# Loading and pooling kv in 8 KB rows with parts of a band matrix, and ten unread products as TensorE's first work

## The chip, the cores and the metric

The kernel runs on one core of a Trainium2 chip. The metric is device time in microseconds (us) of one execution; lower is better. Before the change it takes 1547.98 us, the median of 3 runs (1547.93 to 1549.79).

## What is computed

Three parts follow one another: an attention whose keys and values are a pooled picture, and two feed-forward layers. All data is float32.

```python
B, C, Hh, Ww = (1, 128, 384, 32)             # q: [1, 12288, 128], kv: [1, 384, 32, 128]
kv_pool = kv.reshape(B, H // 4, 4, W // 4, 4, C).mean(axis=(2, 4))
kv_flat = kv_pool.reshape(B, -1, C) @ w_sr   # 768 keys of 128 numbers
k = v = kv_flat
s = (q @ k.transpose(0, 2, 1)) / np.sqrt(C)
a = np.exp(s - s.max(-1, keepdims=True))
a /= a.sum(-1, keepdims=True) + 1e-09
x = (a @ v)
h = x @ w_in1;  x = (np.maximum(h, 0) + alpha * np.minimum(h, 0)) @ w_out1
h = x @ w_in2;  P = a0 + a1*h + a2*h**2 + a3*h**3
Q = 1.0 + abs(b0) * abs(h) + abs(b1) * h**2
out = (P / (Q + 1e-06)) @ w_out2
```

The order of the 768 keys does not matter, as long as keys and values have the same one.

## The kernel before

The work falls into three stages: the **load phase** (kv is loaded and pooled, keys and values are made), the **attention** (24 groups of 512 queries), and the two **layers** (24 groups, 16 blocks of 128 hidden numbers each). Every engine has a program of its own, written out by hand in a fixed order; semaphores tie them together.

**Load phase.** The keys are made in 6 chunks of 128. For each chunk SyncE's queue (SP, L197) issues 4 DMAs of 256 KB. `kv_rows` (L47) puts one 4 x 4 cell of the picture, which is one key, on each partition; of each of its 4 picture rows a partition gets 4 pixels x 128 numbers, that is 2 KB in one piece. A chunk is 16 pixels x 128 numbers on each of the 128 partitions. VectorE sums the first 8 pixels of a chunk (`pool_keys`, one reduction L907 of 1024 numbers to 128 on each partition) as soon as the first two DMAs have landed. TensorE adds up the other 8 pixels by 8 products with the identity (L1363), whose result stands transposed in PSUM, and then adds VectorE's sum with a ninth (L1365). In float32 each such product is recorded as 2 instructions. ScalarE copies the chunk out, divided by 16 (`copy_pooled_t`, L431); TensorE multiplies it with w_sr (`key_chunk`, L1372, and for each three chunks the values, L1376). Two such halves of 384 keys are then split in a high and a low part, by ScalarE (`keys_hi` L437, `values_hi` L442) and VectorE (`keys_lo` L915, `values_lo` L954). The attention's first scores (L1345) wait for the second `keys_lo`.

Between these, TensorE transposes the queries of the first two groups (`queries`, L1404), ScalarE and VectorE split them (`query_hi` L468, `query_lo` L948). After kv, SP issues w_in1 (L199, 1 MB in rows of 8 KB) and w_out1 (L200, 1 MB in pieces of 512 B), and then the queries of each further group when `qt_ready` says that a buffer is free; after three of these it issues w_in2 (L206, 1 MB in rows of 8 KB), which stands in the notes of the profile as in_moe_w_in too.

ScalarE's queue issues at the start w_sr, alpha (8 KB), the coefficients a and b (L423, L424, each given to all 128 partitions, 16 and 8 bytes per partition) and the queries of the first two groups (L426). ScalarE then makes abs(b) (L462). VectorE makes 1 - alpha (L944) after its first reduction, and waits for abs(b) before it. TensorE's first instruction is the transpose of alpha (L1352).

**Attention.** In each step TensorE runs the scores of one group, the transposes of its probabilities and the products with the values (`tile_scores`, `transposed`, `weighted`).

**Entry to the layers.** ScalarE's last piece of the attention is `attended_hi` (L496). It then loads two coefficients into registers and starts `negative(0, 0)` (L552), for whose end TensorE waits with its third block of the first layer.

Of the kernel before, what the change touches and what calls it, by code (L numbers as in the profile page):

```python
# [9 lines left out]
ALU = mybir.AluOpType  # L10
# [3 lines left out]
P = 128  # L14
# [19 lines left out]
def build(nc, q, kv, w_sr, w_in1, w_out1, alpha, w_in2, w_out2, coef_p, coef_q, out):  # L34
# [12 lines left out]
    kv_rows = kv[0].rearrange("(hh r) (ww x) c -> hh ww r (x c)", r=POOL_SIDE, x=POOL_SIDE)  # L47
    key_rows = P // kv_rows.shape[1]
# [4 lines left out]
    with ctx:  # L53
# [48 lines left out]
        pooled = early[:, 0:keys].rearrange("p (c n) -> p c n", c=CHUNKS)  # L102
        w_sr_sb = early[:, keys:keys + P]
        al_rows = early[0:BLOCKS, keys + P:keys + 2 * P]
# [9 lines left out]
        DVE_PIXELS, POOLED, VALUES = 2 * POOL_SIDE, (2, 3, 5, 6, 7, 2), (3, 6)  # L114
# [5 lines left out]
        for name in (  # L120

            *(f"ld_kv{c}{part}" for c in range(CHUNKS) for part in "ab"), "ld_wsr", "ld_in1", "ld_out1", "ld_in2", "ld_out2", "ld_al", "ld_ab", "ld_q0", "ld_q1", "st_out",
# [70 lines left out]
        def _(sp):  # L193

            for c in range(CHUNKS):
                for r in range(POOL_SIDE):
                    sp.dma_start(kv_in[:, c, r * POOL_SIDE * P:(r + 1) * POOL_SIDE * P],  # L197
                                 kv_rows[c * key_rows:(c + 1) * key_rows, :, r, :]).then_inc(s[f"ld_kv{c}{'aabb'[r]}"], 16)
            sp.dma_start(raw_in[0], w_in1).then_inc(s["ld_in1"], 16)  # L199
            sp.dma_start(wout1[:], w_out1.rearrange("(b p) c -> p b c", p=P)).then_inc(s["ld_out1"], 16)  # L200
            for g in range(GROUPS - 2):
                sp.wait_ge(s["qt_ready"], g + 1)
                sp.dma_start(q_in[:, g % 2, :], q_groups[g + 2]).then_inc(s[f"ld_q{g % 2}"], 16)
                if g == 2:
# [213 lines left out]
        def _(act):  # L418
# [122 lines left out]
            act.wait_ge(s["cols_done"], 1)  # L541
# [361 lines left out]
        def _(dve):  # L903
            def pool_keys(c):

                dve.wait_ge(s[f"ld_kv{c}a"], 32)
                nc.vector.tensor_reduce(pooled[:, c, :],  # L907
                                        kv_in[:, c, 0:DVE_PIXELS * P].rearrange("p (j c) -> p c j", j=DVE_PIXELS),
                                        AX.X, ALU.add).then_inc(s["pooled_done"], 1)
# [31 lines left out]
            dve.wait_ge(s["ld_ab"], 32)
            dve.wait_ge(s["absb_col_done"], 1)
            dve.wait_ge(s["al_ready"], 1)
            nc.vector.tensor_scalar(one_minus_al[:], banks[:, 7, 0:BLOCKS], -1.0, 1.0, ALU.mult, ALU.add).then_inc(s["cols_done"], 1)  # L944
# [56 lines left out]
            for g in range(STEPS):  # L1001
# [340 lines left out]
        def _(pe):  # L1342
# [6 lines left out]
            pe.wait_ge(s["ident_ready"], 1)  # L1349

            pe.wait_ge(s["ld_al"], 16)
            nc.tensor.transpose(banks[:, 7, 0:BLOCKS], al_rows, ident[0:BLOCKS, 0:BLOCKS]).then_inc(s["al_ready"], 1)  # L1352

            def pooled_transpose(c):

                dst = banks[:, POOLED[c], 0:P]
# [4 lines left out]
                pe.wait_ge(s[f"ld_kv{c}b"], 32)  # L1361
# [411 lines left out]
```

## Time and profile before

| | us |
|---|---|
| median of 3 runs | 1547.98 |
| the profiled execution | 1547.8 |
| span of its records | 1546.0 |
| TensorE busy, of the span | 1508.4 (98%) |
| VectorE busy | 1433.9 (93%) |
| ScalarE busy | 1401.4 (91%) |
| GpSimd busy | 1230.5 (80%) |

The profiled execution lies 0.2 us under the median of the runs, and 1.8 us of it lie outside the span. PE is TensorE's matmul side, PEld its loading of weights, DVE VectorE, ACT ScalarE, POOL GpSimd, SP SyncE. A "releaser" is what ended an engine's idle time. Times in rows are counted from the start of the span. In the DMA share, 1.00 means that all 16 DMA engines are busy.

### The profile page before, as it was taken

The numbers are of one execution on the slowest core, as the hardware profiler recorded it, in microseconds if no ns is written. First come the engines' busy times: TensorE is split into PE (matmuls) and PEld (weight loads), VectorE is DVE, ScalarE is ACT, GpSimd is POOL, SyncE is SP. The second block draws the span as 40 slices with busy tenths as digits, with TensorE's granted clock in tenths as the row PEclk, the third lists the DMA queues.
The fourth block names the chain that finished last, engine by engine and source line by source line (L and its number), as shares of the span: only waits on it lengthen the run. The fifth ranks groups of instructions, "written<-read, shape, count | busy, mean of one in ns | idle before, by whom it ended". The sixth has DMA issues, their size and how long they took to land. (4 is left out here: it accounts for less than half of the span.)

```text
span 1546.0 us, 28282 instructions
## 1 busy us (share of the span) xinstructions
PE 1508.4 (98%) x8269; PEld 1247.6 (81%) x8269; DVE 1433.9 (93%) x2260; ACT 1401.4 (91%) x2714; POOL 1230.5 (80%) x1346
## 2 busy tenths in 40 slices
PE   6999999999999999999999999999999999999986
PEld 5899999867888888888888888888888888888875
DVE  4788888739999999999999999999999999999998
ACT  1677777749999999999999999999999999999997
POOL 0444444408999999999999999999999999999997
PEclk9999999999999999999999999999999999999998
DMA  8100010000000000000000000000000000000000
GB/s 247 54 24 22 29 48 21 1 1 1 8 8 1 8 8 8 8 1 8 8 8 1 8 8 8 8 1 8 8 8 1 8 8 8 8 1 8 8 8 8
DMA packets 12330, 24.94 MB, mean 16 GB/s; under 512 B 1536, under 2 KB 1680, under 8 KB 11920
## 3 DMA queue, kind: packets, MB, share of 16 engines
q1 hardware_dynamic: 11424, 22.55, 4.7%
q8 instruction: 65, 1.06, 0.3%
q14 instruction: 89, 0.73, 0.1%
q10 hardware_dynamic: 752, 0.60, 0.1%
HBM read 16.85 MB, written 6.29 MB: 15 GB/s over the span
## 5 line engine op out<-in xcount | busy, mean ns | idle before, releaser
L285 POOL TENSOR_TENSOR cubic<-sq,lin_p 128x512 f32<-128x512 f32 x384 | 495.1, 1289 | 75.1 <-ACT sq L560 48.5
L276 POOL TENSOR_TENSOR rational<-newton,ratio 128x512 f32<-128x512 f32 x333 | 429.7, 1291 | 30.8 <-PE banks L1544 21.3
L1544 PEld LDWEIGHTS banks<-wout,rational 128*128 128x128 f32 x3072 | 403.0, 194 | 41.1 <-issue 10.6
L1544 PE MATMUL banks<-wout,rational 128*128 128x128 f32 x3072 | 405.4, 277 | 1.9 <-POOL rational L276 1.4
L1345 PE MATMUL banks<-x_hi,win_lo 128*128 128x512 f32 x768 | 387.8, 505 | 15.0 <-DVE ratio L1054 12.6
L1347 PE MATMUL banks<-x_hi,win_hi 128*128 128x512 f32 x768 | 303.3, 395 | 0.0
L1346 PE MATMUL banks<-x_lo,win_hi 128*128 128x512 f32 x768 | 302.6, 394 | 0.0
L578 ACT ACTIVATE lin_p<-banks,ab_raw 128x512 f32<-128x512 f32 x384 | 294.4, 767 | 3.8 <-PE banks L1347 3.8
L1037 DVE SCALAR_TENSOR_TENSOR banks<-sq,abs_b,banks 128x512 f32<-128x512 f32 x384 | 286.5, 746 | 3.5 <-ACT banks L570 3.1
L1045 DVE SCALAR_TENSOR_TENSOR banks<-banks,ab_raw,cubic 128x512 f32<-128x512 f32 x384 | 287.9, 750 | 0.0
L1054 DVE SCALAR_TENSOR_TENSOR ratio<-banks,ab_raw,rcp 128x512 f32<-128x512 f32 x384 | 285.2, 743 | 1.6 <-POOL rational L276 0.2
L594 ACT ACTIVATE rcp<-log_q 128x512 f32<-128x512 f32 x384 | 277.1, 722 | 0.4
L570 ACT ACTIVATE banks<-banks 128x512 f32<-128x512 f32 x384 | 265.2, 691 | 1.8 <-DVE rational L1072 1.7
L585 ACT ACTIVATE log_q<-banks 128x512 f32<-128x512 f32 x384 | 260.9, 680 | 3.5 <-DVE banks L1037 3.4
L560 ACT ACTIVATE sq<-banks 128x512 f32<-128x512 f32 x384 | 263.2, 686 | 0.2
L1063 DVE SCALAR_TENSOR_TENSOR newton<-banks,rcp 128x512 f32<-128x512 f32 x333 | 224.8, 680 | 1.6 <-ACT rcp L594 1.3
L267 POOL TENSOR_SCALAR newton<-newton 128x512 f32<-128x512 f32 x333 | 207.1, 622 | 20.4 <-DVE newton L1063 13.8
L1345 PEld LDWEIGHTS banks<-x_hi,win_lo 128*128 128x128 f32 x768 | 145.5, 190 | 90.4 <-issue 22.8
L1534 PE MATMUL banks<-neg_part,wout 128*128 128x512 f32 x384 | 196.0, 592 | 0.0
L1346 PEld LDWEIGHTS banks<-x_lo,win_hi 128*128 128x128 f32 x768 | 146.1, 190 | 47.7 <-issue 32.0
L1347 PEld LDWEIGHTS banks<-x_hi,win_hi 128*128 128x128 f32 x768 | 144.6, 188 | 32.9
L485 ACT ACTIVATE pt_hi<-banks 128x512 fp32r<-128x512 f32 x144 | 86.0, 598 | 65.8 <-PE banks L1427 42.9
(91 smaller groups left out, 2305.7 us busy)
## 6 DMA issues: line engine op xcount, KB each, us to landing
early<-in_kv_dram SPq DMA_DIRECT2D x24, 256.0 KB, 9.4
out_dram<-y_out SPq DMA_DIRECT2D x24, 256.0 KB, 2.0
neg_part<-in_q_dram SPq DMA_DIRECT2D x22, 256.0 KB, 2.7
early<-in_moe_w_in_dram SPq DMA_DIRECT2D x1, 1024.0 KB, 14.2
wout<-in_moe_w_in_dram SPq DMA_DIRECT2D x1, 1024.0 KB, 5.3
neg_part<-in_q_dram ACTq DMA_DIRECT2D x2, 256.0 KB, 8.9
early<-in_w_sr_dram ACTq DMA_DIRECT2D x1, 64.0 KB, 2.0
wout<-in_moe_w_out_dram SPq DMA_DIRECT2D x2, 0.5 KB, 12.2
```

The source lines that it names most:

```text
L276: nc.gpsimd.tensor_tensor(rational[:, m % 3, :], newton[:, m % 2, :], ratio[:, m % 2, :], ALU.mult).then_inc(s["rat_done"], 1)
L285: nc.gpsimd.tensor_tensor(cubic[:, m % 2, :], sq[:, m % 2, :], lin_p[:, m % 2, :], ALU.mult).then_inc(s["cubic_done"], 1)
L570: nc.scalar.activation(banks[:, QV[m % 2], :], banks[:, H2[m % 3], :], ACT.Abs, scale=scale_b0).then_inc(s["absb_done"], 1)
L578: nc.scalar.activation(lin_p[:, m % 2, :], banks[:, H2[m % 3], :], ACT.Identity, bias=ab_raw[:, 2:3], scale=scale_a3).then_inc(s["linp_don ...
L594: nc.scalar.activation(rcp[:, m % 2, :], log_q[:, m % 2, :], ACT.Exp, bias=float(-LN_SHIFT * np.log(2.0)), scale=-1.0).then_inc(s["rcp_don ...
L1037: nc.vector.scalar_tensor_tensor(banks[:, QV[m % 2], :], sq[:, m % 2, :], abs_b[:, 1:2], banks[:, QV[m % 2], :], ALU.mult, ALU.add).then_i ...
L1045: nc.vector.scalar_tensor_tensor(banks[:, H2[m % 3], :], banks[:, H2[m % 3], :], ab_raw[:, 1:2], cubic[:, m % 2, :], ALU.mult, ALU.add).th ...
L1054: nc.vector.scalar_tensor_tensor(ratio[:, m % 2, :], banks[:, H2[m % 3], :], ab_raw[:, 0:1], rcp[:, m % 2, :], ALU.add, ALU.mult).then_inc ...
L1345: nc.tensor.matmul(dst, w[1], x[0], start=start, stop=False)
L1346: nc.tensor.matmul(dst, w[0], x[1], start=False, stop=False)
L1347: return nc.tensor.matmul(dst, w[0], x[0], start=False, stop=stop)
L1544: last = nc.tensor.matmul(banks[:, ACC2, t * P:(t + 1) * P], rational[:, m % 3, t * P:(t + 1) * P], wout2[:, c, :], start=(c == 0 and t == ...
```

## The change

kv is read by picture row. A chunk is now 128 picture rows (one on each partition) by 16 pixels: one piece of 8 KB per partition, one DMA of 1 MB per chunk; the first and the last chunk are loaded as two DMAs of 512 KB, in pieces of 4 KB. On a partition lie 4 *units* of 4 neighbouring pixels; a key is the sum over the 4 pixels of a unit and over 4 neighbouring partitions. The sum over partitions is made by TensorE with `spread`, a matrix of 128 x 256 with a band of ones: `row_sums(u)` is a part of it, 128 columns wide, that takes the partitions 4n to 4n+3 to column 32u+n. VectorE sums some of the units over their 4 pixels (512 numbers to 128 on each partition): 2, 2, 3, 3, 2, 2 of the chunks' 4 units, 14 reductions in all. TensorE takes the other 10 units with 4 products each, and VectorE's sums with one each: 54 products in all, as before (6 x 9).

GpSimd clears `spread`, and VectorE writes the band by one reduction of the identity. TensorE's first work is 10 products of the identity with itself into the bank of the transposed queries, which nobody reads. The transpose of alpha moves behind the first chunk.

The queries of the first two groups are issued by SP behind chunks 1 and 2. a and b are issued by SP behind w_out1. ScalarE's abs(b) moves from the start to the entry to the layers, with a wait for it before the registers are loaded. The order of the steps on TensorE, ScalarE and VectorE in the load phase changes so that chunk 1 comes ahead of the first queries.

```diff
-    kv_rows = kv[0].rearrange("(hh r) (ww x) c -> hh ww r (x c)", r=POOL_SIDE, x=POOL_SIDE)
-    key_rows = P // kv_rows.shape[1]
+    kv_rows = kv[0].rearrange("(k h) (n w) c -> k n h (w c)", h=P, n=2)
+    CELLS = P // POOL_SIDE
+    UNITS = P // CELLS
...
+        spread = early[:, 2 * P:4 * P]
+        pooled = early[:, 4 * P:4 * P + CHUNKS * UNITS * P].rearrange("p (c u n) -> p c u n", c=CHUNKS, u=UNITS)
...
+        WARM_UP = 10
+        BY_DVE_UNITS = ((0, 2), (0, 1), (0, 1, 2), (0, 1, 2), (0, 1), (0, 2))
...
-            for c in range(CHUNKS):
-                for r in range(POOL_SIDE):
-                    sp.dma_start(kv_in[:, c, r * POOL_SIDE * P:(r + 1) * POOL_SIDE * P],
-                                 kv_rows[c * key_rows:(c + 1) * key_rows, :, r, :]).then_inc(s[f"ld_kv{c}{'aabb'[r]}"], 16)
+            half = UNITS // 2 * POOL_SIDE * P
+            sp.dma_start(kv_in[:, 0, 0:half], kv_rows[0, 0, :, 0:half]).then_inc(s["ld_kv0"], 16)
+            sp.dma_start(kv_in[:, 0, half:], kv_rows[0, 0, :, half:]).then_inc(s["ld_kv_first"], 16)
+            for c in range(1, CHUNKS - 1):
+                sp.dma_start(kv_in[:, c, :], kv_rows[c // 2, c % 2]).then_inc(s[f"ld_kv{c}"], 16)
+                if c <= 2:
+                    sp.dma_start(q_in[:, c - 1, :], q_groups[c - 1]).then_inc(s[f"ld_q{c - 1}"], 16)
+            sp.dma_start(kv_in[:, CHUNKS - 1, 0:half], kv_rows[CHUNKS // 2 - 1, 1, :, 0:half]).then_inc(s[f"ld_kv{CHUNKS - 1}"], 16)
+            sp.dma_start(kv_in[:, CHUNKS - 1, half:], kv_rows[CHUNKS // 2 - 1, 1, :, half:]).then_inc(s["ld_kv_rest"], 16)
             sp.dma_start(raw_in[0], w_in1).then_inc(s["ld_in1"], 16)
             sp.dma_start(wout1[:], w_out1.rearrange("(b p) c -> p b c", p=P)).then_inc(s["ld_out1"], 16)
+            sp.dma_start(ab_raw[:, 0:4], coef_p.partition_broadcast(P)).then_inc(s["ld_ab"], 16)
+            sp.dma_start(ab_raw[:, 4:6], coef_q.partition_broadcast(P)).then_inc(s["ld_ab"], 16)
...
+            nc.gpsimd.memset(spread, 0.0).then_inc(s["spread0"], 1)
...
-            act.dma_start(ab_raw[:, 0:4], coef_p.partition_broadcast(P)).then_inc(s["ld_ab"], 16)
-            act.dma_start(ab_raw[:, 4:6], coef_q.partition_broadcast(P)).then_inc(s["ld_ab"], 16)
-            for g in (0, 1):
-                act.dma_start(q_in[:, g, :], q_groups[g]).then_inc(s[f"ld_q{g}"], 16)
...
-            act.wait_ge(s["ld_ab"], 32)
-            nc.scalar.activation(abs_b[:], ab_raw[:, 4:6], ACT.Abs).then_inc(s["absb_col_done"], 1)
...
             copy_pooled_t(0)
+            copy_pooled_t(1)
             query_hi(0)
-            copy_pooled_t(1)
+            copy_pooled_t(2)
             query_hi(1)
-            copy_pooled_t(2)
             copy_pooled_t(3)
...
-            act.wait_ge(s["cols_done"], 1)
+            act.wait_ge(s["ld_ab"], 32)
+            nc.scalar.activation(abs_b[:], ab_raw[:, 4:6], ACT.Abs).then_inc(s["absb_col_done"], 1)
+            act.wait_ge(s["absb_col_done"], 1)
...
-                dve.wait_ge(s[f"ld_kv{c}a"], 32)
-                nc.vector.tensor_reduce(pooled[:, c, :],
-                                        kv_in[:, c, 0:DVE_PIXELS * P].rearrange("p (j c) -> p c j", j=DVE_PIXELS),
-                                        AX.X, ALU.add).then_inc(s["pooled_done"], 1)
+                dve.wait_ge(s[f"ld_kv{c}"], 16)
+                for u in BY_DVE_UNITS[c]:
+                    if c == 0 and u >= UNITS // 2:
+                        dve.wait_ge(s["ld_kv_first"], 16)
+                    if c == CHUNKS - 1 and u >= UNITS // 2:
+                        dve.wait_ge(s["ld_kv_rest"], 16)
+                    pixels = kv_in[:, c, u * POOL_SIDE * P:(u + 1) * POOL_SIDE * P]
+                    nc.vector.tensor_reduce(pooled[:, c, u, :], pixels.rearrange("p (x n) -> p n x", x=POOL_SIDE),
+                                            AX.X, ALU.add).then_inc(s["pooled_done"], 1)
...
+            nc.vector.tensor_reduce(spread[:, P - CELLS:P], ident[:].rearrange("p (n r) -> p n r", r=POOL_SIDE),
+                                    AX.X, ALU.add).then_inc(s["row_sums_done"], 1)
...
             pool_keys(1)
+            dve.wait_ge(s["al_ready"], 1)
+            nc.vector.tensor_scalar(one_minus_al[:], banks[:, 7, 0:BLOCKS], -1.0, 1.0, ALU.mult, ALU.add).then_inc(s["cols_done"], 1)
+            pool_keys(2)
             query_lo(0)
-            pool_keys(2)
+            pool_keys(3)
             query_lo(1)
-            pool_keys(3)
             pool_keys(4)
...
+            for n in range(WARM_UP):
+                nc.tensor.matmul(banks[:, Q_T, 0:P], ident[:], ident[:], start=(n == 0), stop=(n == WARM_UP - 1))
...
+            def row_sums(u):
+                first = P - CELLS - u * CELLS
+                return spread[:, first:first + P]
...
-                for j in range(DVE_PIXELS, PIXELS):
-                    nc.tensor.matmul(dst, kv_in[:, c, j * P:(j + 1) * P], ident[:], start=(j == DVE_PIXELS), stop=False)
-                pe.wait_ge(s["pooled_done"], c + 1)
-                nc.tensor.matmul(dst, pooled[:, c, :], ident[:], start=False, stop=True).then_inc(s["pooled_t_ready"], 1)
+                for u in by_pe:
...
+                    for x in range(POOL_SIDE):
+                        at = (u * POOL_SIDE + x) * P
+                        nc.tensor.matmul(banks[:, POOLED[c], 0:P], kv_in[:, c, at:at + P], row_sums(u),
+                                         start=(u == by_pe[0] and x == 0), stop=False)
+                for n, u in enumerate(BY_DVE_UNITS[c]):
+                    pe.wait_ge(s["pooled_done"], made_before + n + 1)
+                    last = nc.tensor.matmul(banks[:, POOLED[c], 0:P], pooled[:, c, u, :], row_sums(u),
+                                            start=False, stop=(n == len(BY_DVE_UNITS[c]) - 1))
+                last.then_inc(s["pooled_t_ready"], 1)
...
             pooled_transpose(0)
+            turn_alpha()
+            pooled_transpose(1)
+            key_chunk(0)
             queries(0)
-            pooled_transpose(1)
-            queries(1)
-            key_chunk(0)
             pooled_transpose(2)
             key_chunk(1)
+            queries(1)
```

## Rows read from the trace of the kernel before

**Rows 1.** Busy time by stretch, with TensorE's granted clock, DMA share and rate

```profile
core 0: us, PE busy (x) PEld busy (x) DVE busy (x) ACT busy (x) POOL busy (x), PEclk, DMA share, GB/s
2.00:4.00 2.00, 0.00 (x0) 0.00 (x0) 0.00 (x0) 0.02 (x1) 0.00 (x0) 1.00 0.86 248
4.00:8.00 4.00, 0.25 (x1) 0.18 (x1) 1.87 (x1) 0.00 (x0) 0.00 (x0) 1.00 0.55 132
8.00:28.00 20.00, 15.17 (x110) 14.60 (x111) 9.90 (x9) 2.94 (x8) 0.00 (x0) 1.00 1.07 298
44.50:46.00 1.50, 1.50 (x12) 1.49 (x11) 1.04 (x3) 0.56 (x3) 0.74 (x4) 1.00 1.04 415
60.00:290.00 230.00, 230.00 (x1404) 208.96 (x1403) 190.42 (x334) 169.74 (x330) 106.24 (x241) 1.00 0.09 26
```

**Rows 2.** Waits of TensorE, then VectorE, in 0 to 34 us: total, times, longest

```profile
PE banks L1363 <- DMA early<-in_kv_dram: 9.4, 5, 6.0
...
DVE early L907 <- DMA early<-in_kv_dram: 13.7, 6, 5.8
```

**Rows 3.** Timeline: start, us, engine, line, operation, count [idle before <- releaser]

```profile
18.86 2.05 PE L1363 MATMUL banks<-ident,early 128*128 128x128 f32 x16 [0.59 <-DMA early<-in_kv_dram]
20.75 0.39 PE L1365 MATMUL banks<-ident,early 128*128 128x128 f32 x2
...
24.72 0.83 PE L1376 MATMUL banks<-early,wout 128*128 128x128 f32 x6
...
29.80 2.02 PE L1363 MATMUL banks<-ident,early 128*128 128x128 f32 x16 [1.33 <-DMA early<-in_kv_dram]
...
31.89 1.02 PE L1372 MATMUL banks<-wout,early 128*128 128x128 f32 x4
34.08 0.44 PE L1345 MATMUL banks<-k_hi,q_lo 128*128 128x384 f32 x1 [0.50 <-DVE k_lo L915]
...
41.17 0.60 PE L1404 MATMUL banks<-ident,neg_part 128*128 128x128 f32 x4
```

**Rows 4.** DMA packets and queues of the stretch 4 to 5 us

```profile
DMA packets 160, 0.09 MB, mean 94 GB/s; under 512 B 115, under 2 KB 115, under 8 KB 160
...
q10 hardware_dynamic: 103, 0.00, 5.3%
```

**Rows 5.** Issues: count, KB each, us from issue to landing

```profile
neg_part<-in_q_dram SPq DMA_DIRECT2D x1, 256.0 KB, 18.0
...
wout<-in_moe_w_in_dram SPq DMA_DIRECT2D x1, 1024.0 KB, 5.3
...
ab_raw<-in_moe_a_dram ACTq DMA_DIRECT2D x1, 2.0 KB, 4.3
ab_raw<-in_moe_b_dram ACTq DMA_DIRECT2D x1, 1.0 KB, 6.9
```

**Rows 6.** VectorE's groups by form in 0 to 345 us: busy, mean ns

```profile
L963 DVE TENSOR_REDUCE neg_max<-banks 128x1 f32<-128x768 f32 x96 | 91.5, 953 | 27.2 <-PE banks L1347 27.2
...
L948 DVE TENSOR_TENSOR q_lo<-banks,q_hi 128x512 fp32r<-128x512 f32 x24 | 16.5, 687 | 3.2 <-ACT q_hi L468 2.1
...
L907 DVE TENSOR_REDUCE early<-early 128x128 f32<-128x1024 f32 x6 | 11.4, 1903 | 13.7 <-DMA early<-in_kv_dram 13.7
...
L982 DVE TENSOR_TENSOR wout_lo<-wout,wout_hi 128x1024 fp32r<-128x1024 f32 x1 | 1.2, 1215 | 0.0
```

**Rows 7.** Timeline of TensorE's first float32 products

```profile
10.77 3.78 PE L1363 MATMUL banks<-ident,early 128*128 128x128 f32 x16 [6.00 <-DMA early<-in_kv_dram]
14.35 0.64 PE L1365 MATMUL banks<-ident,early 128*128 128x128 f32 x2
```

**Rows 8.** Timeline at the entry to the layers, with abs(b) of the start (first row)

```profile
9.14 0.20 ACT L462 ACTIVATE abs_b<-ab_raw 128x2 f32<-128x2 f32 x1 [7.12 <-DMA ab_raw<-in_moe_b_dram]
...
320.93 0.60 ACT L552 ACTIVATE neg_part<-banks 128x512 f32<-128x512 f32 x1 [0.24 <-PE banks L1347]
...
321.58 0.19 PEld L1345 LDWEIGHTS banks<-x_hi,win_lo 128*128 128x128 f32 x1 [0.57 <-ACT neg_part L552]
```

More of the change, by code:

```diff
@@ L100, in build @@
         w_in1_t = early[:, tokens // 2 + ff:tokens // 2 + 2 * ff].rearrange("p (b c) -> p b c", b=BLOCKS)
-        pooled = early[:, 0:keys].rearrange("p (c n) -> p c n", c=CHUNKS)
-        w_sr_sb = early[:, keys:keys + P]
-        al_rows = early[0:BLOCKS, keys + P:keys + 2 * P]
+        w_sr_sb = early[:, 0:P]
+        al_rows = early[0:BLOCKS, P:2 * P]
+        spread = early[:, 2 * P:4 * P]
+        pooled = early[:, 4 * P:4 * P + CHUNKS * UNITS * P].rearrange("p (c u n) -> p c u n", c=CHUNKS, u=UNITS)
         q_in = neg_part
@@ L112, in scores @@
             return banks[:, 2 * n:2 * n + 2, 0:HALF]
-        DVE_PIXELS, POOLED, VALUES = 2 * POOL_SIDE, (2, 3, 5, 6, 7, 2), (3, 6)
+        WARM_UP = 10
+        BY_DVE_UNITS = ((0, 2), (0, 1), (0, 1, 2), (0, 1, 2), (0, 1), (0, 2))
+        POOLED, VALUES = (2, 3, 5, 6, 7, 2), (3, 6)
         Q_T, P_T, ATT = 4, (5, 6), 7
@@ L120, in build @@
         for name in (
-            *(f"ld_kv{c}{part}" for c in range(CHUNKS) for part in "ab"), "ld_wsr", "ld_in1", "ld_out1", "ld_in2", "ld_out2", "ld_al", "ld_ab", "ld_q0", "ld_q1", "st_out",
+            *(f"ld_kv{c}" for c in range(CHUNKS)), "ld_kv_first", "ld_kv_rest", "spread0", "row_sums_done", "ld_wsr", "ld_in1", "ld_out1", "ld_in2", "ld_out2", "ld_al", "ld_ab", "ld_q0", "ld_q1", "st_out",
             "ident0", "absb_col_done", "al_ready", "ident_ready", "pooled_done", "pooled_t_ready", "pooled_t_copied", "k_ready", "k_hi_done", "k_lo_done",
@@ L937, in scale_out1 @@
                                         ALU.mult).then_inc(s["out1_scaled"], 1)
+            dve.wait_ge(s["ident_ready"], 1)
+            dve.wait_ge(s["spread0"], 1)
+            nc.vector.tensor_reduce(spread[:, P - CELLS:P], ident[:].rearrange("p (n r) -> p n r", r=POOL_SIDE),
+                                    AX.X, ALU.add).then_inc(s["row_sums_done"], 1)
             pool_keys(0)
[L941 to L944, printed above, removed]
             def query_lo(g):
@@ L1030, in _ @@
                     scale_out1(g - SCALE_STEP)
+            dve.wait_ge(s["ld_ab"], 32)
+            dve.wait_ge(s["absb_col_done"], 1)
             def denominator(g, c):
@@ L1349, in _, with turn_alpha @@
             pe.wait_ge(s["ident_ready"], 1)
-            pe.wait_ge(s["ld_al"], 16)
-            nc.tensor.transpose(banks[:, 7, 0:BLOCKS], al_rows, ident[0:BLOCKS, 0:BLOCKS]).then_inc(s["al_ready"], 1)
+            for n in range(WARM_UP):
+                nc.tensor.matmul(banks[:, Q_T, 0:P], ident[:], ident[:], start=(n == 0), stop=(n == WARM_UP - 1))
+            def turn_alpha():
+                pe.wait_ge(s["ld_al"], 16)
+                nc.tensor.transpose(banks[:, 7, 0:BLOCKS], al_rows, ident[0:BLOCKS, 0:BLOCKS]).then_inc(s["al_ready"], 1)
+            def row_sums(u):
+                first = P - CELLS - u * CELLS
+                return spread[:, first:first + P]
             def pooled_transpose(c):
-                dst = banks[:, POOLED[c], 0:P]
+                by_pe = [u for u in range(UNITS) if u not in BY_DVE_UNITS[c]]
+                made_before = sum(len(units) for units in BY_DVE_UNITS[:c])
                 if c == 4:
@@ L1360, in pooled_transpose @@
                     pe.wait_ge(s["pooled_t_copied"], 1)
-                pe.wait_ge(s[f"ld_kv{c}b"], 32)
-                for j in range(DVE_PIXELS, PIXELS):
-                    nc.tensor.matmul(dst, kv_in[:, c, j * P:(j + 1) * P], ident[:], start=(j == DVE_PIXELS), stop=False)
-                pe.wait_ge(s["pooled_done"], c + 1)
-                nc.tensor.matmul(dst, pooled[:, c, :], ident[:], start=False, stop=True).then_inc(s["pooled_t_ready"], 1)
+                pe.wait_ge(s[f"ld_kv{c}"], 16)
+                if c == 0:
+                    pe.wait_ge(s["row_sums_done"], 1)
+                for u in by_pe:
+                    if c == 0 and u >= UNITS // 2:
+                        pe.wait_ge(s["ld_kv_first"], 16)
+                    if c == CHUNKS - 1 and u >= UNITS // 2:
+                        pe.wait_ge(s["ld_kv_rest"], 16)
+                    for x in range(POOL_SIDE):
[7 more added lines that the diff above has]
+                last.then_inc(s["pooled_t_ready"], 1)
             def key_chunk(c):
```

## The prediction

> **What bounds the kernel now.** I read the busy time by stretch first. From 60 to 290 us TensorE is busy without a gap [rows 1], so the attention takes as long as TensorE needs, and whatever the load phase gives or takes shifts all of it, and the layers behind it, one for one. The change leaves the products of both alone. What counts is therefore when the attention's first score starts, 34.08 us [rows 3], and one edit at the entry to the layers.
>
> Next I read who waits in the load phase. TensorE waits 9.4 us in 5 stops for kv, and VectorE 13.7 us in 6 [rows 2]; two of TensorE's stops are 0.59 and 1.33 us long, ahead of chunk 2 at 18.86 and ahead of chunk 5 at 29.80 us [rows 3]. So kv's arrival sets the pace. The chain from it is short: the last quarter of kv releases TensorE at 29.80, the last sum is taken in and TensorE turns to its product with w_sr at 31.89, and 2.2 us later (copy, product, high part, low part) the scores start at 34.08 [rows 3]. That end of the chain is the same after the change. I compare the point of 31.89.
>
> Why does kv come slowly? From 8 to 28 us the DMA engines are full (share 1.07) and move 298 GB/s in pieces of 2 KB. From 44.5 to 46 us, while w_in2 comes in rows of 8 KB, they are as full (1.04) and move 415 GB/s [rows 1]. And from 4 to 8 us they move only 132 GB/s at a share of 0.55 [rows 1]: of 160 packets between 4 and 5 us 115 are under 512 B, and 103 are on ScalarE's queue [rows 4]. The pieces of a and b, of 16 and 8 bytes, stand in kv's way; their landing takes 4.3 and 6.9 us [rows 5].
>
> **The change part by part.**
>
> *Arrival.* Up to the last piece of kv come 6.29 MB of kv, 0.52 MB of queries and some 0.07 MB of w_sr and alpha: 6.89 MB. w_in2, 1.05 MB, lands 5.3 us after its issue [rows 5]. At 375 GB/s 2.8 us of this are movement and 2.5 are fixed. For the rate I take 375 and not 415, for the 5.3 us contain slower first and last parts; ends are 298 (nothing gained) and 415. SP's first issue stands at 0.7 us, and 0.2 us are for the shared start: a piece lands at 3.4 us plus its cumulated bytes by 0.375 MB per us. The tiny packets are gone from this stretch. That gives chunk 0 at 5.0 and 6.4 us, chunk 1 at 9.2, chunk 2 at 12.7, chunk 3 at 16.2, chunk 4 at 19.0, and chunk 5 at 20.4 and 21.8, where the last piece before came at 29.80. (At the 248 GB/s of 2 to 4 us [rows 1] the first half of chunk 0 would land at 5.8; nothing waits for it that long, as shown below.) About 8 us are there to be had, if the engines keep up.
>
> The Trainium skill speaks against this part: "DMA: Bandwidth & Descriptors", Specifications, has transfers at line rate from 512 B on, so that pieces of 2 KB would already be as good as pieces of 8 KB. By that rule the rate would stay at its level and only the tiny packets would give something; the trace disagrees with its 298 against 415 GB/s at the same share.
>
> *VectorE.* 6 reductions of 1024 numbers become 14 of 512, with the same stride. One of 1024 takes 1.90 us [rows 6]. What is the fixed part of a VectorE instruction? Subtractions of 512 and 1024 numbers take 0.687 and 1.215 us, so 1.03 ns a number and 0.16 us fixed; by that 768 numbers make 0.95 us, which is what the maximum over 768 contiguous numbers takes [rows 6]. The pooling reduction has 1.90 - 0.16 = 1.74 us beside the fixed part, where 1024 numbers at 1.03 ns make 1.06. If all of it goes with the numbers read, a unit costs 0.16 + 0.87 = 1.03 us. If the excess of 0.68 goes with the 128 results, it costs 0.16 + 0.53 + 0.68 = 1.37. Below, half of 1.90 is 0.95. I take 1.03, since the maximum at full speed differs from the pooling above all in that it reads neighbours, the pooling at steps of 512 bytes; 1.37 is a rival. The sum is 14.4 us against 11.4.
>
> The Trainium skill bears on that choice: "SBUF — State Buffer", Door 1, says that fp32 reads with a step beyond a 16-byte line pay a penalty for each access, which would be a cost by number read. By it the unit costs 1.03, by results 1.37; no row tells them apart.
>
> *TensorE.* 54 pooling products stay 54. Eight take 1.89 us (18.86 to 20.75), so 0.24 each [rows 3]. The ten unread products run at the slow pace: TensorE's first 16 instructions of this kind took 3.58 us to the next start (10.77 to 14.35) [rows 7], 0.45 per product, twice the later price. The granted clock stands at 1.00 in all of these rows, so the profile does not show the level by that column, only by the durations; after about 4 us of work the engine is at the fast pace. Ten cost 4.5 us, from about 1.9 to 6.4 us, when nothing else is there to do: chunk 0 lands at 5.0, so 1.4 us of it are past the first landing, given back by chunk 0's eight products at 1.9 instead of 3.6 us. On the path both are worth nothing, since waits for chunks 1 and 2 come behind.
>
> *Sum.* VectorE starts chunk 2 at 12.7: three units to 15.8, `query_lo` 0.69 [rows 6] to 16.5, chunk 3 to 19.6. TensorE waits for that, takes the last sum in by 19.9, and is the later one from here: a key product 0.23 and the values of the first half 0.83 [rows 3] to 20.9, chunk 4's eight products 1.9 and two for VectorE's sums 0.45 to 23.3, a key product 0.23, chunk 5's ten to 25.8. VectorE has its last unit at 24.9. So 31.89 becomes 25.8: 6.1 us less.
>
> *Entry to the layers.* abs(b) took 0.20 us at the start. Now it stands between `attended_hi` and `negative(0, 0)`, with a semaphore's round trip behind it. ScalarE's gap there is 0.24 us (the registers), and TensorE waits 0.57 us for `negative` [rows 8], so nothing hides it: 0.20 + about 0.15 = 0.35 us more, bounds 0.2 and 0.6. VectorE's new wait for it has `negative_lo` behind it, which waits for ScalarE's next piece anyway.
>
> *At nothing:* clearing `spread` and making the band (GpSimd and VectorE idle until the first landing); the alpha transpose. SP now issues 10 DMAs ahead of w_in1 in place of 24; a and b stand behind w_out1 and ahead of group 2's queries. These took 18.0 us to land before [rows 5]. Now 2.1 MB and the tiny packets come behind 21.8: w_in1 at 375 GB/s 2.8 us, w_out1 in its small pieces at 298 3.5, and for a and b the 4 us of the slow stretch [rows 1], so some 32.5 us with their own 0.7; TensorE took them at 41.17 [rows 3] and wants them near 35. If the cover of some 2 us is gone, the excess is paid.
>
> Net 6.1 - 0.35 = 5.75 us: the profiled execution 1547.8 becomes 1542.05, and its 0.2 us under the median makes **1542.2 us**.
>
> **The rivals.**
> - *Reductions cost by result (1.37 us).* VectorE: chunk 2 to 16.8, 17.5, chunk 3 to 21.6, 22.3, chunk 4 to 25.0, `keys_lo` 25.5, chunk 5 to 28.3, TensorE's product 28.5. Gain 3.4 - 0.35: 1544.9 us. For it: VectorE has more to do than before, and this is its only price without a row.
> - *The rate stays at 298.* Chunk 3 lands at 19.6 and the last piece at 26.8 us; TensorE's ten of chunk 5 end at 28.9. Gain 3.0 - 0.35: 1545.3. Against it is the 415 row; for it, that kv's rows lie 16 KB apart in memory while w_in2 is contiguous. Both rivals together: 1547.4.
> - *TensorE stays at the slow pace.* If the gaps before chunks 2 and 3 (up to 2 us) keep it there, all 54 products cost 0.45: TensorE's own sum is 6.4 + 24.3 + 4.5 for keys, values and queries = 35.2 us, and 0.7 more behind it: 4.0 + 0.35 slower, **1552.3 us**. It decides from some 27 slow products on (6.1 by 0.22). Against it: gaps of 1.33 us and a load of the same density kept the pace before [rows 3].
> - *It does less than it says:* the new load is no better, but tiny packets are gone: that is the second rival.
>
> **How the numbers follow.** Forecast 0.63; by result 0.14; rate 0.08; both 0.04; slow pace 0.04; 0.07 for a faster course (415 GB/s and 0.95 us: 7.4 us gained, 1540.6) or a late queue. The range reaches from 1540.5 to 1545.4. A measurement of this kernel can tell about 0.2% (3.1 us) from no change, so faster means under 1544.9. The forecast, the fast course and half of the first rival lie there: 0.77. Within 0.2%: the other half, the rate, both: 0.18. Slower: 0.05.
>
> **What would show it.** Right: first score near 28.0 us; DMA rate of 350 or more from 6 to 20 us with no tiny packets; units of 1.03 us; TensorE's wait for chunk 3's sums; an `abs_b` row near 320 us less the shift, and a wait of about 0.9 us behind. Wrong: units of 1.3 us, a rate near 300, or pooling products of 0.45 us after chunk 0.

## The result

| | before | after |
|---|---|---|
| median of 6 runs, us | 1549.14 (1547.93 to 1550.4) | 1540.14 (1539.6 to 1541.57) |
| ratio after / before | | 0.9942, 95% interval 0.9931 to 0.9952 |
| profiled execution, us | 1547.8 | 1539.87 |
| span of its records, us | 1546.0 | 1538.1 |

The kernel became faster by 0.58%, that is 9.0 us (7.4 to 10.7). The two profiled executions differ by 7.9 us. The median of before was 1547.98 us in the first three runs and is 1549.14 in six; 1.2 us of the distance between 5.8 forecast and 9.0 measured is that. Forecast was 1542.2 us in a range from 1540.5 to 1545.4; 1540.14 lies 0.4 us outside, on the fast side; that is less than the six runs of the changed kernel differ among themselves (2.0 us).

### The profile page after: what moved, and what is told of

Its sections match the earlier page's. It is cut to its first block and busy times, and to the rows that moved or that the text cites. A ratio compares the mean times of both kernels' runs of the same rounds, so it can differ in the third digit from the quotient of the medians.

```text
span 1538.1 us, 28317 instructions
## 1 busy us (share of the span) xinstructions
PE 1509.9 (98%) x8289; PEld 1250.0 (81%) x8289; DVE 1435.8 (93%) x2269; ACT 1401.1 (91%) x2714; POOL 1230.8 (80%) x1347
## 3 DMA queue, kind: packets, MB, share of 16 engines
q8 instruction: 65, 1.06, 0.3%
```

## The profile after

Busy time by stretch of the changed kernel (columns as in [rows 1]):

```profile
core 0: us, PE busy (x) PEld busy (x) DVE busy (x) ACT busy (x) POOL busy (x), PEclk, DMA share, GB/s
2.00:4.00 2.00, 2.00 (x10) 2.00 (x11) 0.11 (x1) 0.02 (x1) 0.00 (x0) 1.00 0.87 297
4.00:8.00 4.00, 4.00 (x24) 4.00 (x24) 2.06 (x2) 0.00 (x0) 0.00 (x0) 1.00 1.01 410
8.00:20.00 12.00, 10.60 (x84) 9.56 (x84) 10.22 (x13) 2.74 (x7) 0.00 (x0) 1.00 1.03 423
...
54.00:284.00 230.00, 230.00 (x1406) 209.06 (x1405) 190.68 (x333) 169.79 (x329) 106.60 (x242) 1.00 0.09 26
```

Against [rows 1]: the slow stretch of 4 to 8 us is gone (410 in place of 132 GB/s), the steady rate is 423 in place of 298 at about the same DMA share, and the attention is the same wall of TensorE work. Its timeline in the load phase:

```profile
1.85 4.64 PE L1367 MATMUL banks<-ident 128*128 128x128 f32 x20 [1.85 <-POOL ident L234]
...
6.28 2.37 PE L1396 MATMUL banks<-early 128*128 128x128 f32 x16
...
9.19 2.05 PE L1396 MATMUL banks<-early 128*128 128x128 f32 x16
...
11.85 2.93 DVE L920 TENSOR_REDUCE early<-early 128x128 f32<-128x512 f32 x3 [1.08 <-DMA early<-in_kv_dram]
...
14.83 0.49 PE L1400 MATMUL banks<-early 128*128 128x128 f32 x2 [0.45 <-DVE early L920]
...
15.30 2.92 DVE L920 TENSOR_REDUCE early<-early 128x128 f32<-128x512 f32 x3
...
18.27 0.49 PE L1400 MATMUL banks<-early 128*128 128x128 f32 x2 [0.45 <-DVE early L920]
...
24.18 1.02 PE L1409 MATMUL banks<-wout,early 128*128 128x128 f32 x4
...
26.37 0.44 PE L1361 MATMUL banks<-k_hi,q_lo 128*128 128x384 f32 x1 [0.50 <-DVE k_lo L927]
```

The point that the prediction compares, TensorE's last products with w_sr, moved from 31.89 to 24.18 us, and the first score from 34.08 [rows 3] to 26.37, 7.7 us earlier. TensorE no longer waits for kv at all. What it waits for is VectorE (waits of TensorE, then of VectorE: total, times, longest; compare [rows 2]):

```profile
PE banks L1400 <- DVE early L920: 1.3, 3, 0.4
```

```profile
DVE early L920 <- DMA early<-in_kv_dram: 5.6, 4, 2.4
```

VectorE waits four times, last for chunk 2 at 11.85; chunk 3's units run from 15.30 without a wait. From chunk 2 on the path is VectorE's, from 18.27 on TensorE's; how little ahead of VectorE kv is by then, e6 shows below.

The entry to the layers, timeline: `x_hi` before, which [rows 8] leave out, and then the kernel after:

```profile
320.09 0.60 ACT L496 ACTIVATE x_hi<-banks 128x512 fp32r<-128x512 f32 x1 [1.78 <-PE banks L1347]
```

```profile
312.37 0.60 ACT L501 ACTIVATE x_hi<-banks 128x512 fp32r<-128x512 f32 x1 [1.78 <-PE banks L1363]
...
312.86 0.20 ACT L547 ACTIVATE abs_b<-ab_raw 128x2 f32<-128x2 f32 x1
...
313.92 0.60 ACT L559 ACTIVATE neg_part<-banks 128x512 f32<-128x512 f32 x1 [0.86 <-ACT abs_b L547]
...
314.57 0.50 PE L1361 MATMUL banks<-x_hi,win_lo 128*128 128x512 f32 x1 [0.85 <-ACT neg_part L559]
```

Before, the third block started at 321.58 [rows 8], 1.49 us behind `x_hi`; now it is 2.20. So 0.7 us are given back here.

**Where the rest is.** The start of `y_out` marks the end of each of the 24 groups of the second layer. The first of them, before and after:

```profile
406.20 0.68 DVE L1101 TENSOR_SCALAR y_out<-banks 128x512 f32<-128x512 f32 x1
```

```profile
399.15 0.68 DVE L1117 TENSOR_SCALAR y_out<-banks 128x512 f32<-128x512 f32 x1
```

The distance is 7.05 us there, 7.26 at the 22nd group (1448.99 and 1441.73), and then 7.76 and 7.86 at the last two. So the changes of the load phase and the entry (7.7 - 0.7) arrive at the layers' end almost whole, and some 0.6 us come only in the last two groups. There single executions scatter: against the kernel before, one of the runs below gains 2.2 us in them (e12_gap_8k: 3.01 behind at the 22nd group, 0.78 at the last), one gains 0.9 (e4_before_ab_moved: 1.07 ahead, then 2.02) and one loses 0.9 (e5_abs_mid: 7.72 ahead, then 6.79). The granted clock there is below full (0.79 before and 0.82 after from 1490 to 1538 us, 1.00 and 0.99 in the ninety us ahead of that). I count these 0.6 us to no edit. In what follows the first score is the measure of the load phase; it is read from one execution of each kernel, and scatters too: e5_abs_mid does the same work as the kernel after up to there, and its first score is 0.25 us earlier.

## The experiments

Two questions stand: what made kv come so fast, and what each smaller edit is worth.

**e1_no_products: the ten unread products.**

```diff
-            for n in range(WARM_UP):
-                nc.tensor.matmul(banks[:, Q_T, 0:P], ident[:], ident[:], start=(n == 0), stop=(n == WARM_UP - 1))
```

> The changed kernel without its ten unread products. In its trace the first score starts at 26.37 us, 7.71 before that of the kernel before. Theory (arrival theory): the products are worth nothing on the path; TensorE starts chunk 0 at 4.6 us at the slow pace, ends it near 9.0 instead of 9.1, and the first score stays at 26.4, at most 0.4 later. Rival (pace theory): the fast pace from chunk 0 on is a real part of the gain; chunks 0 and 1 cost up to 2 us more and the first score comes at 27.5 to 28.4.

Measured: 1540.54 us, ratio 0.9949 (0.9932 to 0.9965), first score at 26.63. TensorE starts chunk 0 at the slow pace and is still in time:

```profile
4.63 3.48 PE L1394 MATMUL banks<-early 128*128 128x128 f32 x16 [4.63 <-DMA early<-in_kv_dram]
...
9.00 2.05 PE L1394 MATMUL banks<-early 128*128 128x128 f32 x16 [0.28 <-DMA early<-in_kv_dram]
```

Eight products took 3.3 us to the next start at 7.95, but they began 1.65 us earlier, and chunk 1 was waited for anyway. The first score is 0.26 us later, about the scatter of one execution, so the ten products are worth 0.3 us at most there and nothing that the times can tell.

**e2_ab_first and e4_before_ab_moved: the tiny packets, put back into the kernel after and taken out of the kernel before.**

```diff
+            act.dma_start(ab_raw[:, 0:4], coef_p.partition_broadcast(P)).then_inc(s["ld_ab"], 16)
+            act.dma_start(ab_raw[:, 4:6], coef_q.partition_broadcast(P)).then_inc(s["ld_ab"], 16)
...
-            sp.dma_start(ab_raw[:, 0:4], coef_p.partition_broadcast(P)).then_inc(s["ld_ab"], 16)
-            sp.dma_start(ab_raw[:, 4:6], coef_q.partition_broadcast(P)).then_inc(s["ld_ab"], 16)
```

The lines are e2's. e4 moves the two DMAs the other way and, since abs(b) needs them, makes it in step 8 of the attention.

> The changed kernel, but a and b are issued by ScalarE's queue at the start again (the queries stay on SP). Theory: their 256 tiny packets take the DMA engines from kv between 3 and 8 us as before, where 132 GB/s were moved in place of 298; some 2 us of arrival are lost, of which chunk 2 and 3 wait for about 1.5: first score at 27.5 to 28.5. Rival (piece theory, all of the gain is the 8 KB): first score at 26.4 to 26.7.

> The kernel before with one part of the change alone: a and b are issued by SP behind w_out1, and abs(b) is made by ScalarE in step 8 of the attention. Theory: 4 to 8 us are moved at 298 instead of 132 GB/s, so kv lands 2.2 us earlier and the first score starts at 31.6 to 32.2 instead of 34.08; the time falls by 1.9 to 2.5 us. Rival (piece theory): nothing, 34.0.

Measured: e2 1542.85 us, ratio 0.9957 (0.9941 to 0.9974), first score at 28.51, 2.1 us later than in the kernel after. e4 1546.89 us, ratio 0.9985 (0.9976 to 0.9995), first score at 32.84, 1.2 us earlier than in the kernel before. The stretches of e2 show the hole that the tiny packets make, here from 6 to 10 us:

```profile
4.00:6.00 2.00, 2.00 (x11) 2.00 (x11) 1.27 (x2) 0.00 (x0) 0.00 (x0) 1.00 1.05 403
6.00:8.00 2.00, 2.00 (x13) 2.00 (x12) 0.80 (x1) 0.00 (x0) 0.00 (x0) 1.00 0.83 279
8.00:9.00 1.00, 1.00 (x12) 1.00 (x11) 0.00 (x0) 0.00 (x0) 0.00 (x0) 1.00 0.55 138
9.00:10.00 1.00, 0.74 (x7) 0.52 (x6) 0.25 (x1) 0.28 (x1) 0.00 (x0) 1.00 0.41 123
```

In the kernel after the packets cost the upper end of what the theory said (2.1 us, 1.1 to 2.1 expected), in the kernel before, by the first score, less than expected (1.2 us in place of 2.2; the times alone, 2.3 us apart with an interval from 0.8 to 3.7, can't tell). From 4 to 8 us e4 moves 289 GB/s in place of 132, as the theory said, but from 8 to 20 us 284 in place of 298. By an estimate from these rates, 14 GB/s less up to 20 us and 11 less up to 28 us (289 against 300) make 0.26 MB, or 0.9 us, which is about what is missing; why the rate is lower there is not shown. The packets are one part of the gain, not most of it.

**e3_pieces_2k and e7_pieces_4k: the size of the pieces.** The same places in the same order, but 24 DMAs with pieces of 2 KB, or 12 with 4 KB.

```diff
-                sp.dma_start(kv_in[:, c, :], kv_rows[c // 2, c % 2]).then_inc(s[f"ld_kv{c}"], 16)
+                for at in range(0, UNITS * POOL_SIDE * P, piece_n):
+                    sp.dma_start(kv_in[:, c, at:at + piece_n], kv_rows[c // 2, c % 2, :, at:at + piece_n]).then_inc(s[name], 16)
```

> The changed kernel, but kv comes in 24 DMAs of 256 KB in pieces of 2 KB again, to the same places and in the same order. Theory: the rate falls from 423 to about 300 GB/s from 8 to 20 us, the last piece lands near 26.5, the first score starts near 30 (29.2 to 30.8), 3 to 4.5 us later than in the changed kernel. Rival (packet theory: what mattered was the tiny packets, 2 KB are at line rate): first score at 26.4 to 27.0.

> The changed kernel with kv in 12 DMAs of 512 KB, in pieces of 4 KB, the partitions in one run as in the changed kernel. 2 KB pieces in that form moved 388 GB/s from 8 to 20 us (e3_pieces_2k), 8 KB 423. Form theory (what is slow is the 16 x 8 form of the source, the piece size is a small term): 400 to 420 GB/s here, first score at 26.4 to 27.2. Rival (a threshold above 4 KB): 385 to 392 GB/s, first score at 27.8.

Measured: e3 1542.34 us, ratio 0.9958 (0.9942 to 0.9975), first score at 27.81; e7 1539.54 us in one run, first score at 26.16. Stretch 8 to 20 us of e3, then of e7:

```profile
8.00:20.00 12.00, 9.16 (x66) 7.68 (x66) 8.79 (x11) 2.03 (x5) 0.00 (x0) 1.00 1.05 388
```

```profile
8.00:20.00 12.00, 10.60 (x82) 9.43 (x82) 10.42 (x13) 2.74 (x7) 0.00 (x0) 1.00 1.04 413
```

This felled my theory: with pieces of 2 KB I had expected 300 GB/s and got 388. The size of the pieces is worth 35 GB/s and 1.4 us; something else in the new load is worth 90. What differs is how the source is walked. `kv_rows` before is a pattern of two steps over the partitions, 16 groups of 8 (16 x 8 from here on); after the change the 128 partitions are one run with one step. And the addresses differ with it: 8 neighbouring pieces and then a jump of 64 KB, against pieces 16 KB apart. (In e3 and e7 the size of one DMA shrinks with the piece, 256 and 512 KB in place of 1 MB; the two are not told apart.)

**e8, e9, e11, e10, e12: form of the source or addresses.** All change only the source of kv in the kernel after. In e8, e11 and e12 other pixels meet in a key than the reference's; their traces are read, not their output. In e9 and e10 only the order of the keys changes (the expectation of e9 says otherwise, wrongly: four neighbouring partitions still hold four neighbouring picture rows).

```diff
+ e8:  kv[0].rearrange("(i j) (y w) c -> i (j y) (w c)", i=24, w=4)              # one run, 2 KB, no gaps
+ e9:  kv[0].rearrange("(a g b) (y w) c -> g y a b (w c)", a=16, g=3, w=4)       # 16 x 8, 2 KB
+ e11: kv[0].rearrange("(h k) (n w) c -> k n h (w c)", h=P, n=2)                 # one run, 8 KB, 48 KB apart
+ e10: kv[0].rearrange("(a g b) (n w) c -> g n a b (w c)", a=16, g=3, n=2)       # 16 x 8, 8 KB
+ e12: kv[0][120*k:120*k+144].rearrange("(a g) (n w) c -> n a g (w c)", g=9, n=2)[:, :, 0:8, :]   # 16 x 8, 8 KB, every ninth row skipped
```

> As e3_pieces_2k (24 DMAs of 256 KB in 2 KB pieces), but each DMA reads 256 KB that lie in one piece in memory, partition after partition; the pooled sums are then of other pixels, so the output is not the attention's. In e3 the pieces lie 16 KB apart and the rate from 8 to 20 us was 388 GB/s; in the kernel before they lie in 16 groups of 8 neighbours, the groups 64 KB apart, and it was 298. Address theory: neighbouring 2 KB pieces are slow, so 280 to 310 GB/s here. Shape theory (the 16 x 8 form of the source is what is slow): 370 to 400 GB/s here.

> As e3_pieces_2k, but each DMA reads 16 groups of 8 pieces: the pieces of a group lie 16 KB apart as in e3, the groups 384 KB apart, so that the source has the form 16 x 8 of the kernel before without its neighbouring pieces; the pooled sums are of other pixels. Shape theory: 280 to 310 GB/s from 8 to 20 us, first score near 30. Address theory: 370 to 400 GB/s, first score as in e3, 27.8.

> The changed kernel, 8 KB pieces and 1 MB per DMA, but the source of each kv DMA has the form 16 x 8: 16 groups of 8 neighbouring picture rows, the groups 24 rows apart. The keys are the same in another order. Form theory, first kind (the form spreads the partitions badly over the DMA engines, whatever the piece): 270 to 330 GB/s from 8 to 20 us, first score at 29 to 31.5. Form theory, second kind (the form costs something per piece, so that 2 KB pieces suffer most): 390 to 425 GB/s, first score at 26.3 to 27.

> The changed kernel, but the picture rows of a chunk lie 48 KB apart in memory in place of 16 KB, at one step (the partitions remain one run); the pooled sums are of other pixels, so the output is not the reference's. Form theory: as in the changed kernel, 415 to 425 GB/s from 8 to 20 us, first score at 26.1 to 26.7. Address theory (what is slow in the kernel before, and in e9 and e10, is that the pieces lie in groups far apart): below 350 GB/s, first score after 28.

> As e10_split_8k, but the groups of 8 picture rows are 9 rows apart in place of 24: the addresses are almost those of the changed kernel (every ninth row is skipped), while the source still has the form 16 x 8. Some rows of kv are then not read and others twice, so the output is not the reference's. Form theory: as e10, 220 to 300 GB/s from 8 to 20 us, first score at 32 to 39. Address theory: 410 to 425 GB/s, first score at 26.1 to 26.7.

Measured, one run each (GB/s from 8 to 20 us; the kernels before and after for comparison):

| kernel | form | piece | addresses | GB/s | first score |
|---|---|---|---|---|---|
| after | one run | 8 KB (ends 4 KB) | 16 KB apart | 423 | 26.37 |
| e11_far_8k | one run | 8 KB | 48 KB apart | 421 | 26.41 |
| e7_pieces_4k | one run | 4 KB | 16 KB apart | 413 | 26.16 |
| e8_flat_2k | one run | 2 KB | neighbours | 393 | 27.07 |
| e3_pieces_2k | one run | 2 KB | 16 KB apart | 388 | 27.81 |
| before | 16 x 8 | 2 KB | 8 neighbours, then 64 KB | 298 | 34.08 |
| e4_before_ab_moved | 16 x 8 | 2 KB | as before | 284 | 32.84 |
| e9_split_2k | 16 x 8 | 2 KB | 16 KB, then 384 KB | 271 | 33.33 |
| e12_gap_8k | 16 x 8 | 8 KB | 16 KB, every ninth skipped | 236 | 36.67 |
| e10_split_8k | 16 x 8 | 8 KB | 16 KB, then 384 KB | 232 | 38.01 |

The stretch 8 to 20 us of e11, e8, e9, e12 and e10, whose rows carry this:

```profile
8.00:20.00 12.00, 10.79 (x86) 9.74 (x86) 10.19 (x13) 2.74 (x7) 0.00 (x0) 1.00 1.03 421
```

```profile
8.00:20.00 12.00, 9.72 (x72) 8.23 (x71) 9.54 (x12) 2.54 (x7) 0.00 (x0) 1.00 1.06 393
```

```profile
8.00:20.00 12.00, 7.11 (x52) 6.16 (x52) 6.21 (x8) 1.15 (x3) 0.00 (x0) 1.00 1.06 271
```

```profile
8.00:20.00 12.00, 7.94 (x50) 7.17 (x50) 5.00 (x7) 1.15 (x3) 0.00 (x0) 0.86 1.02 236
```

```profile
8.00:20.00 12.00, 8.04 (x49) 7.36 (x49) 4.61 (x6) 1.15 (x3) 0.00 (x0) 0.86 1.03 232
```

The form decides, over all sizes and addresses tried: no 16 x 8 source passes 298 GB/s, no source in one run falls under 388. e12 is the sharp one: its addresses are the changed kernel's but for every ninth row, and it moves 236 GB/s in place of 423. e11 shows that wide steps alone cost nothing, e8 and e3 that neighbours or not matters little. It is not a cost per piece either, for with four times fewer pieces the form is slower still (232 and 236 against 271); both of e10's ranges were missed, and e9's 271 and 33.33 us lie on the slow side of "280 to 310" and "near 30".

Nor does the form cut the pieces smaller. SP's queue from 8 to 20 us in the kernel after and in e12 (packets, MB, share of the 16 engines' time):

```profile
q1 hardware_dynamic: 1001, 5.06, 102.1%
```

```profile
q1 hardware_dynamic: 601, 2.83, 101.6%
```

A packet has 5.1 KB on average in the one and 4.7 KB in the other, but it holds its engine for 0.20 us in the one and 0.32 in the other (the share of 16 x 12 us, divided by the packets). So packets of about the same size take longer.

By what way the form does this is not shown. The Trainium skill ("DMA: Bandwidth & Descriptors", The descriptor swizzle) describes for a 128-partition transfer that each DMA engine writes the partitions of one port of SBUF. That a 16 x 8 form loses this order would fit, but no run here separates it from other ways.

e9 also prices the form by the first score: with all other edits in place and without the tiny packets it has 33.33 us, against 27.81 of e3, so 5.5 us for the form, at 2 KB. So with a 16 x 8 form and pieces of 2 KB the rest of the change brings 0.75 us in the load phase and loses 0.7 at the entry. With the source left just as it was it might bring more, since e9's addresses give 271 GB/s and those of the kernel before 298; no run has that.

In e10 and e12 TensorE's granted clock falls as well. Timeline of e10, ahead of chunk 1 and at chunk 3, and its stretch 20 to 28 us:

```profile
12.97 3.68 PE L1397 MATMUL banks<-early 128*128 128x128 f32 x16 [3.12 <-DMA early<-in_kv_dram]
...
24.09 2.08 PE L1397 MATMUL banks<-early 128*128 128x128 f32 x8 [1.31 <-DMA early<-in_kv_dram]
```

```profile
20.00:28.00 8.00, 5.78 (x27) 4.83 (x27) 5.52 (x7) 1.00 (x3) 0.00 (x0) 0.71 0.98 217
```

After a wait of 3.12 us eight products take 3.5 us to the next start (12.97 to 16.45) in place of 1.9, and later, at a mean clock of 0.71, four take 1.9 (24.09 to 25.96). That is the lower of the two levels (1.2 in place of 2.4 GHz) for part of the stretch. It adds to a load that is late anyway. In e9, whose stops for kv are up to 2.2 us long, the eight products behind that stop take 1.9 us.

**e5_abs_mid: abs(b) at the entry.**

```diff
+                if g == 8:
+                    act.wait_ge(s["ld_ab"], 32)
+                    nc.scalar.activation(abs_b[:], ab_raw[:, 4:6], ACT.Abs).then_inc(s["absb_col_done"], 1)
...
-            act.wait_ge(s["ld_ab"], 32)
-            nc.scalar.activation(abs_b[:], ab_raw[:, 4:6], ACT.Abs).then_inc(s["absb_col_done"], 1)
             act.wait_ge(s["absb_col_done"], 1)
```

> The changed kernel, but ScalarE makes abs(b) in step 8 of the attention; the registers are loaded where they were. Theory (entry theory): in the changed kernel the wait for abs(b) lets the register loads start only behind it, and TensorE waits 0.85 us for the first neg_part instead of 0.57; with abs(b) early ScalarE's gap is 0.24 us again and the distance from x_hi to the third block of the first layer is 0.7 us shorter, 0.5 to 0.8 us of the time. Rival: the 0.7 us come from elsewhere (code loading, another order of waits), and the distance stays.

Measured: 1539.84 us, ratio 0.9934 (0.9922 to 0.9947), beside 0.9942 of the kernel after; the intervals overlap. The trace is clear:

```profile
312.13 0.60 ACT L501 ACTIVATE x_hi<-banks 128x512 fp32r<-128x512 f32 x1 [1.78 <-PE banks L1364]
...
312.97 0.60 ACT L560 ACTIVATE neg_part<-banks 128x512 f32<-128x512 f32 x1 [0.24 <-PE banks L1364]
...
313.62 0.50 PE L1362 MATMUL banks<-x_hi,win_lo 128*128 128x512 f32 x1 [0.15 <-ACT neg_part L560]
```

From `x_hi` to the third block 1.49 us, as before the change. Of the 0.7 us, 0.09 are abs(b) itself, which ended at 313.06 where `x_hi` had ended at 312.97; ScalarE's gap ahead of `neg_part` was 0.86 and is 0.24, so nearly all of it is what lay behind the wait for abs(b): the semaphore's way back and the register loads. The loads have no rows of their own, and no run separates the two; that the loads run beside `x_hi` when no wait holds them back is inferred from the gap.

**e6_units: what bounds the load phase now.** e5, and VectorE sums two units of chunk 2 in place of three.

```diff
-        BY_DVE_UNITS = ((0, 2), (0, 1), (0, 1, 2), (0, 1, 2), (0, 1), (0, 2))
+        BY_DVE_UNITS = ((0, 2), (0, 1), (0, 1), (0, 1, 2), (0, 1), (0, 2))
```

> As e5_abs_mid, and VectorE sums 2 units of chunk 2 in place of 3 (TensorE takes the third with 4 products for one: 3 more in all). Theory (the path now runs over VectorE's sums of chunks 2 and 3, then TensorE): VectorE is done with chunk 3 a unit (0.97 us) earlier, TensorE loses its stops of 0.43 and 0.45 us in chunk 2 for 0.7 us of products; first score 0.1 to 0.5 us earlier than 26.37. Rival (arrival is the bound): first score unchanged within 0.1; a third, TensorE alone is the bound: 0.3 to 0.7 later.

Measured: 1538.8 us, ratio 0.9931 (0.9918 to 0.9944); first score at 26.05, 0.3 us before the kernel after, but only 0.07 before e5 (26.12), which has the old units and differs from the kernel after by 0.25 already in the load phase, where the two do the same work. So one unit moved is worth nothing beyond that scatter. TensorE's stops for VectorE fall from 1.3 to 0.9 us, and the three more products take them up. And VectorE, a unit ahead, has to wait for kv again, at chunk 3:

```profile
14.99 2.91 DVE L921 TENSOR_REDUCE early<-early 128x128 f32<-128x512 f32 x3 [0.55 <-DMA early<-in_kv_dram]
```

In e5 it starts chunk 3 at 15.04 without a wait, so of the 0.97 us that the moved unit frees it keeps 0.05 (0.24 of the rest is that chunk 2 came at 11.85, in e5 at 11.61). Against e5 the expectation's rival (arrival is the bound, unchanged within 0.1) is what happened, and its theory is not borne out. kv's arrival, VectorE and TensorE are close to level; TensorE alone, the third, is not the bound either. It is the fastest kernel by its median; against the kernel after its interval overlaps.

## Why the prediction was wrong, by its steps

- **What bounds the kernel, and the carry-over: right.** The shift at the first score, 7.7 us, less the entry's 0.7 us, is at the 22nd of 24 groups still 7.26.
- **Arrival: wrong in size and in its cause.** This is the step that failed. The rate was taken as 375 GB/s, the fixed part of one 1 MB load being spread over it; it was 423, above even the upper end of 415. VectorE began chunk 2 at 11.85 in place of 12.7 and chunk 3 at 15.30 in place of 16.5. And the cause was read wrongly: two rows that differ in piece size and in the form of the source (kv 298, w_in2 415) were put down to the piece size. The form is most of it, the piece size 35 GB/s. That the gain had the right sign and came out near the forecast is luck, for the change happened to alter both; e10 has the large pieces with the old form, where the prediction would have seen a gain, and its first score is at 38.01, 3.9 us later than before. This step is most of the miss, but alone it does not reach past the range: with 7.7 us at the first score in place of 6.1, and 0.7 at the entry in place of 0.35, the prediction's own sum gives 1541.0. The other 0.9 us to the time measured are 0.3 us between the entry and the 22nd group and 0.6 us in the last two groups, and no edit explains them.
- **The rule of the Trainium skill that I set aside** ("DMA: Bandwidth & Descriptors", Specifications: line rate from 512 B on) was nearer to this chip, for pieces of 2 KB, than my reading: 388 GB/s with 2 KB is not the rate of 8 KB, but far from the 298 that I held against the rule. With pieces of 512 B the trace goes against it. From 22 to 24 us of the changed kernel comes almost nothing but w_out1, in such pieces and with its partitions in one run:

```profile
22.00:24.00 2.00, 2.00 (x20) 2.00 (x20) 1.57 (x3) 0.58 (x2) 0.00 (x0) 1.00 1.05 296
```

  These are 296 GB/s at a share of 1.05. No run changes this load's pieces alone, so it is a row and not a price.
- **Tiny packets: right in kind.** They cost 2.1 us in the kernel after and 1.2 in the kernel before; the sum has no term of its own for them.
- **VectorE's unit: right.** 14 reductions have a mean of 1.03 us (13.9 us busy), the price by numbers read; following each other they start every 0.97 us, 0.06 less than I counted for each. The rival of 1.37 us is out.
- **TensorE and the ten products: right.** 4.4 us from 1.85 to 6.28, chunk 0's eight products 2.2 in place of 1.9, chunk 1's 1.9, and nothing that the times can tell on the path; e1 has 0.3 us in the first score.
- **The sum:** 25.8 was forecast for the last product, it was 24.18. Of these 1.6 us, 0.85 are there at VectorE's start of chunk 2 (arrival), 1.3 by 18.27, where TensorE takes chunk 3's last sum in place of 19.6, and the last 0.3 come in TensorE's steps behind it. The 0.5 in the middle are shorter steps of VectorE: three units and `query_lo` take 3.45 us from 11.85 to 15.30 where the sum has 3.8, and the next three 3.0 in place of 3.1.
- **Entry to the layers: right in place and sign, half in size.** 0.35 us with an upper bound of 0.6 were given, 0.7 measured. The row was misread: the gap of 0.24 us was put down to the registers, but the row names TensorE's block as what ended it (0.24 <-PE banks L1347 [rows 8]), so it tells nothing of them. The new wait uncovered a gap of 0.86 us for them and the semaphore (e5).
- **The rivals.** The rate at 298 was priced at 3.0 us of gain before the entry (by its own terms, 3.4 + 6.89 / 0.298, the last piece lands at 26.5 and not 26.8, so 3.3); e9, whose rate is 271, shows 0.75. The slow pace did not come in the changed kernel: TensorE never stops for a chunk there, and its longest stop for a sum is 0.45 us. It comes in e10 and e12, behind stops of 3.1 and 2.8 us, so the rival had the right place and the wrong load.
- **The queue behind a and b: right in that nothing is paid, wrong in time.** b, the later of the two, landed at 27.5 us (issued at 23.7, 3.8 to the landing) in place of 32.5 (its terms add up to 32.8). w_out1 had landed at 27.0 where the sum has 28.1, and b 0.5 us behind it where the sum has 4.7: behind the bulk load the tiny packets cost almost nothing. TensorE transposed group 2's queries at 33.45 without a stop.

## What to carry to other kernels

Where a load is slow at a full DMA share, look at how its source walks over the partitions before its piece size: a source that gives the 128 partitions one step moved 388 to 423 GB/s here with any piece from 2 to 8 KB and any addresses tried, one of 16 groups of 8 at most 298. Two rows of a trace that differ in two things don't price either; ask which other row has only one of them. And a wait set before a piece of work also uncovers the register loads behind it: put small preparations of a stage some steps ahead of its entry. Here that brought 0.7 us at the entry, which the times of the whole kernel don't tell from nothing.

## What was not expected of the hardware

- The form of a DMA's source alone, at nearly the same addresses and the same 8 KB pieces, took the rate from 423 to 236 GB/s (e12), and larger pieces made the slow form slower (232 and 236 against 271 GB/s), all at a DMA share of 1.02 to 1.06: the share tells that the engines are occupied, not that they move data well.
- 256 packets of 16 and 8 bytes on a second queue brought the DMA engines from 403 to 123 GB/s in e2, at a share of 0.41: the engines stood partly idle, though SP had kv waiting in its queue.
- In e10 the granted clock column shows the lower level (0.71 as a mean of 8 us), while it stands at 1.00 over the first products of before, after and e1, which took just as long (0.42 to 0.45 us each, where later ones take 0.23). In the first microseconds only the durations tell.
